# Causal masks taken off TensorE, and the order of a head's products redone, in a kernel of attention and two routed expert layers

## What is computed

```python
scores = scale * np.matmul(q, k.transpose(0, 1, 3, 2))
cum = np.cumsum(np.log(np.clip(f, 0.0001, 1.0)), axis=-1)
decay = cum[:, :, :, None] - cum[:, :, None, :]
causal = np.triu(np.ones((S, S), dtype=bool), k=1)
scores = np.where(causal, -1000000000.0, scores + decay)
scores = scores - np.max(scores, axis=-1, keepdims=True)
attn = np.exp(scores)
attn = attn / (np.sum(attn, axis=-1, keepdims=True) + 1e-09)
return np.matmul(attn, v)
```

## Time and profile before

| | us |
|---|---|
| three executions, median | 980.33 |
| lowest, highest of the three | 976.04, 981.48 |
| the profiled execution | 977.94 |
| its span | 976.4 |
| TensorE busy in the span | 905.9 |
| VectorE, ScalarE, Pool busy in the span | 554.5, 403.2, 229.0 |

### The profile page before, as it was taken

How to read it: one execution, slowest core, us unless ns; L and a number is a source line. 1 busy time by engine, 2 the same in 40 slices (tenths; PEclk the granted TensorE clock), 3 DMA queues, 4 the chain that set the end, 5 groups by cost and what they waited for, 6 DMA issues and landing times.

```text
span 976.4 us, 16405 instructions
## 1 busy us (share of the span) xinstructions
PE 905.9 (93%) x5244; PEld 727.0 (74%) x5245; DVE 554.5 (57%) x1524; ACT 403.2 (41%) x708; POOL 229.0 (23%) x287
## 2 busy tenths in 40 slices
PE   3999999999988859999999999995999999999996
PEld 3777677677666648888888888874888888888885
DVE  7565567557647526757567776752666243626633
ACT  1344444444445405525435543420555242525532
POOL 3111121321311242322232332313122212222211
PEclk9899999999979969999999999996999999999998
DMA  2334333444423019526254555421666124616110
GB/s 74 106 98 115 101 88 111 121 130 133 116 83 107 26 57 320 175 91 210 66 175 137 172 179 174 143 88 33 207 207 215 44 82 165 202 42 209 44 33 22
DMA packets 59242, 119.64 MB, mean 123 GB/s; under 512 B 11934, under 2 KB 20638, under 8 KB 59204
## 3 DMA queue, kind: packets, MB, share of 16 engines
q1 hardware_dynamic: 49476, 96.90, 31.5%
q0 software_dynamic: 9440, 22.18, 7.0%
q10 hardware_dynamic: 288, 0.07, 0.0%
HBM read 104.14 MB, written 17.99 MB: 125 GB/s over the span
## 4 chain that ended last, share of the span: by engine, by line
PE 86%; ACT 4%; DVE 4%; issue 2%; DMA 2%; POOL 1%; POOLq 0%; SPq 0%; DVEq 0%; ACTq 0%
PE ps L583 25%; PE ps L554 25%; PE ps L411 7%; PE ps L424 7%; PE ps L419 4%; PE ps L374 3%; PE ps L377 3%; PE ps L391 3%; PE ps L392 2%; PE ps L429 2%; ACT qB L626 2%; PE ps L379 1%; PE ps L401 1%; PE ps L395 1%; ACT o_rows L634 1%
## 5 line engine op out<-in xcount | busy, mean ns | idle before, releaser
L971 DVE TENSOR_TENSOR wlo<-stage,whi 128x1024 fp32r<-128x1024 f32 x136 | 160.0, 1221 | 35.7 <-ACT whi L651 34.1
L651 ACT CAST whi<-stage 128x1024 fp32r<-128x1024 f32 x136 | 133.7, 1056 | 0.1
L715 ACT ACTIVATE h_s<-ps 128x512 f32<-128x512 f32 x44 | 26.3, 599 | 224.1 <-PE ps L554 224.1
L620 ACT ACTIVATE probT<-ps 128x576 f32<-128x576 f32 (+4 forms) x160 | 66.2, 434 | 124.2 <-PE ps L395 111.4
L411 PE MATMUL ps<-probT,v_s 128*65 128x448 f32 (+4 forms) x384 | 111.1, 400 | 0.0
L554 PE MATMUL ps<-whi,xT_hi 128*128 128x512 f32 x352 | 96.9, 398 | 3.0 <-DVE xT_lo L1025 3.0
L583 PE MATMUL ps<-whi,hT_hi 128*128 128x512 f32 x352 | 99.5, 404 | 0.0
L583 PE MATMUL ps<-whi,hT_lo 128*128 128x512 f32 x352 | 99.2, 403 | 0.0
L554 PE MATMUL ps<-wlo,xT_hi 128*128 128x512 f32 x352 | 96.4, 396 | 0.0
L554 PE MATMUL ps<-whi,xT_lo 128*128 128x512 f32 x352 | 96.2, 396 | 0.0
L583 PE MATMUL ps<-wlo,hT_hi 128*128 128x512 f32 x352 | 94.9, 391 | 0.0
(11 more groups left out here) (175 smaller groups left out, 1566.0 us busy)
## 6 DMA issues: line engine op xcount, KB each, us to landing
stage<-in_moe_w SPq DMA_DIRECT2D x128, 512.0 KB, 3.8
q_raw<-in_q SPq DMA_DIRECT2D x64, 144.0 KB, 3.0
k_raw<-in_k SPq DMA_DIRECT2D x64, 144.0 KB, 3.1
v_s<-in_v SPq DMA_DIRECT2D x32, 162.5 KB, 2.3
x<-o_rows SPq DMA_DIRECT2D x8, 512.0 KB
kB<-cum_hl SPq DMA_DIRECT2D x64, 2.2 KB, 1.7
table<-entry POOLq DMA_INDIRECT x44, 2.1
table<-tinit SPq DMA_DIRECT2D x2, 288.0 KB
```

Of the source, the lines that this page charges most:

```text
L620: act.activation(probT[0:M, PT_AT[t]:PT_AT[t] + S - t * P], ps[0:M, T_AT[t]:T_AT[t] + S - t * P], ACT.Exp, scale=-1.0).then_inc(exps_done, 1)
L651: act.copy(whi[b][:, c, :], stage[:, c, :]).then_inc(w_hi[c], 1)
L971: dve.tensor_tensor(wlo[b][:, c, :], stage[:, c, :], whi[b][:, c, :].bitcast(F32), ALU.subtract).then_inc(w_lo[c], 1)
```

## The change

The query side's mask goes into the minimum: `tensor_reduce` becomes `tensor_tensor_reduce`, which adds a slice of a 128x576 float32 tile `maskf` (zero but for a triangle of 1e9 at its end) to the scores in PSUM, writes the sum back in place and gives the minimum as its accumulator. The key side's mask is dropped from TensorE; behind each exponential Pool sets the part above the diagonal of the block of `probT` to zero (`clear`, five selects per head), and `weighted` waits for `cleared` in place of `exps_done`. The orders of TensorE, VectorE, ScalarE and Pool within a head are rewritten. SyncE's list is not touched.

```diff
 def by_query(h, j):
-    diag = lo <= q0 < hi
-    ... identb[:], maskb[:, 0:M] ...
+    pe.matmul(o, qB..., kB..., start=True, stop=False)
+    mm = pe.matmul(o, qA..., kA..., start=False, stop=True)
 for h in range(HEADS):                      # TensorE
                 by_key(h, 0)
                 by_key(h, 1)
-                if h > 0:
-                    pe.wait_ge(ot_done, h)
-                    pe.wait_ge(s_embn, 3)
-                    back(h - 1)
                 if more:
                     operands(n)
                     by_query(n, 4)
                 pe.wait_ge(exps_done, QT * h + 1)
                 by_key(h, 2)
+                    by_query(n, 3)
                 pe.wait_ge(v_in[h % 3], (h // 3 + 1) * 16)
+                if h > 0:
+                    pe.wait_ge(ot_done, h)
+                pe.wait_ge(cleared, QT * h + 1)
                 weighted(h, 0)
                 by_key(h, 3)
                     by_query(n, 2)
                 pe.wait_ge(exps_done, QT * h + 2)
-                weighted(h, 1)
                 by_key(h, 4)
                     by_query(n, 1)
                     by_query(n, 0)
-                pe.wait_ge(exps_done, QT * h + 3)
-                weighted(h, 2)
+                pe.wait_ge(cleared, QT * h + 2)
+                weighted(h, 1)
+                if h > 0:
+                    back(h - 1)
                     minima_row(n)
+                weighted(h, 2)
+                weighted(h, 3)
+                weighted(h, 4)
                 if h % H == 6 and h > H:
+                    pe.wait_ge(norm_done, h)
                     g_ranks(h // H - 1)
-                weighted(h, 3)
-                weighted(h, 4)
 def mins(h, j):
-                dve.tensor_reduce(smin[0:q1 - q0, j:j + 1], ps[0:q1 - q0, S_AT[j]:S_AT[j] + q1], AX.X, ALU.min)
+                tile = ps[0:M, S_AT[j]:S_AT[j] + q1]
+                dve.tensor_tensor_reduce(out=tile, in0=tile, in1=maskf[0:M, at:at + q1], scale=1.0, scalar=LARGE,
+                                         op0=ALU.add, op1=ALU.min, accum_out=smin[0:M, j:j + 1])
 for h in range(HEADS):                      # VectorE
-                if h > 0:
-                    norm(h - 1)
-                    mins(n, 4)
                     leading_k(m)
+                    mins(n, 4)
                     mins(n, 3)
+                    rest_k(m)
                     mins(n, 2)
-                    rest_q(m)
                     mins(n, 1)
                     mins(n, 0)
-                    rest_k(m)
+                    rest_q(m)
+                    norm(h - 1)
+def clear(h, t):                            # Pool
+    block = probT[0:M, PT_AT[t]:PT_AT[t] + M]
+    pool.wait_ge(exps_done, QT * h + t + 1)
+    pool.affine_select(out=block, in_=block, compare_op=ALU.is_ge, fill=0.0, ...).then_inc(cleared, 1)
 for h in range(HEADS):                      # Pool
-                    copies(h + 2)
+                    copy_k(h + 2)
+                clear(h, 0)
+                clear(h, 1)
+                clear(h, 2)
+                    copy_q(h + 2)
+                clear(h, 3)
+                clear(h, 4)
```

More of the change, by code:

```diff
@@ L16 @@
 MASKED = 1.0e9
+LARGE = 3.0e38
 OOB = 1 << 20
-S_PASSES = 2
 def attention_moe_moe(nc, q_t, k_t, v_p, f, emb_t, tau, w1a, w2a, wg, w1b, w2b, out):
@@ L133, in attention_moe_moe @@
         probT = asb("probT", [P, PT_AT[-1] + LR])
+        maskf = asb("maskf", [P, S])
         smin = asb("smin", [P, QT], F32R)
@@ L489, in _ @@
                 by_key(h, 2)
+                if more:
+                    if h == 0:
+                        pe.wait_ge(s_embn, 1)
+                    if h > 1:
+                        pe.wait_ge(norm_done, h - 1)
+                if h % H == 7 and h > H:
+                    pe.wait_ge(rank_read, h // H)
+                if more:
+                    by_query(n, 3)
                 pe.wait_ge(v_in[h % 3], (h // 3 + 1) * 16)
+                if h > 0:
+                    pe.wait_ge(ot_done, h)
+                pe.wait_ge(cleared, QT * h + 1)
                 weighted(h, 0)
@@ L493, in _ @@
                 if more:
-                    if h > 0:
-                        pe.wait_ge(norm_done, h)
-                    by_query(n, 3)
                     pe.wait_ge(mins_done, QT * n + 1)
@@ L505, in _ @@
                     by_query(n, 0)
-                pe.wait_ge(exps_done, QT * h + 3)
-                weighted(h, 2)
+                pe.wait_ge(cleared, QT * h + 2)
+                weighted(h, 1)
+                if h > 0:
+                    if more:
+                        pe.wait_ge(mins_done, QT * (n + 1))
+                    pe.wait_ge(s_embn, 3)
+                    if h > 1:
+                        pe.wait_ge(norm_done, h - 1)
+                    back(h - 1)
                 if more:
@@ L817, in mins @@
                 q0, q1 = Q_TILES[j]
-                dve.tensor_reduce(smin[0:q1 - q0, j:j + 1], ps[0:q1 - q0, S_AT[j]:S_AT[j] + q1], AX.X,
-                                  ALU.min).then_inc(mins_done, 1)
+                M = q1 - q0
+                tile = ps[0:M, S_AT[j]:S_AT[j] + q1]
+                at = S - P + M - q1
+                dve.tensor_tensor_reduce(out=tile, in0=tile, in1=maskf[0:M, at:at + q1], scale=1.0, scalar=LARGE, op0=ALU.add,
+                                         op1=ALU.min, accum_out=smin[0:M, j:j + 1]).then_inc(mins_done, 1)
             def embeddings():
@@ L1111, in _, with copy_q, copy_k @@
             pool.sem_inc(s_pool, 1)
-            def copies(h):
-                a = h % 3
+            def copy_q(h):
                 pool.wait_ge(q_hi, h + 1)
-                pool.tensor_copy(qB[a][0:D, :], qA[a][0:D, :].bitcast(F32)).then_inc(q_cp, 1)
+                pool.tensor_copy(qB[h % 3][0:D, :], qA[h % 3][0:D, :].bitcast(F32)).then_inc(q_cp, 1)
+            def copy_k(h):
                 pool.wait_ge(k_hi, h + 1)
-                pool.tensor_copy(kB[a][0:D, 0:S], kA[a][0:D, 0:S].bitcast(F32)).then_inc(k_cp, 1)
-            copies(0)
-            copies(1)
+                pool.tensor_copy(kB[h % 3][0:D, 0:S], kA[h % 3][0:D, 0:S].bitcast(F32)).then_inc(k_cp, 1)
+            def clear(h, t):
+                M = min(P, S - t * P)
+                block = probT[0:M, PT_AT[t]:PT_AT[t] + M]
+                pool.wait_ge(exps_done, QT * h + t + 1)
+                pool.affine_select(out=block, in_=block, compare_op=ALU.is_ge, fill=0.0, base=0, pattern=[[1, M]],
+                                   channel_multiplier=-1).then_inc(cleared, 1)
+            for h in range(2):
+                copy_q(h)
+                copy_k(h)
             pool.iota(tok_i[:], pattern=[[S, B], [P, QT]], base=0, channel_multiplier=1)
```

41 lines of the change are left out of this document (14 added, 27 removed).

## The result

| | before | after |
|---|---|---|
| median of four executions, us | 979.23 | 1004.02 |
| lowest, highest | 976.04, 981.48 | 998.8, 1007.07 |
| the profiled execution, its span | 977.94, 976.4 | 998.8, 997.2 |
| mean granted clock in it | 0.964 | 0.934 |

The changed kernel is slower: the ratio is 1.024, with a 95% interval of 1.0199 to 1.0281. The forecast was 1014 us and slower, with a range of 988 to 1040.

What follows compares the result with a forecast made beforehand. TensorE's own instruction list, with its waits, was taken to bound the attention. Terms -28.5 + 37.1 + 17.5 + 5.7 + 6 - 3.5 = +34.3 on 977.9 gave 1012, 1014 us against the median; range 988 to 1040.

Steps and rivals of the forecast that it cites:

- the seven waits: TensorE before weighted 0 at h = 4, 8, ..., 28: late store delays k's load; 7 x 5.3 = +37.1 us.
- plain heads: TensorE, attention heads without special work: 8.97 us falls to 8.05 (7.9 to 8.3); 31 x 0.92 = -28.5 us.
- the clock behind them: TensorE after each 5.3 us idle: half clock for 3 to 6.8 us; 7 x 2.5 = +17.5 us.
- routing and its clock: Iteration ends at hh = 5 and 6: choose_batch and ranks come later; +5.7 us, plus +6 for lowered clock.
- squares, last batch: Heads behind squares wait about 0.4 instead of 0.68; two dear last-batch heads stay near 13 us; together -3.5.
- the mask's price: Ten mask matmuls per head on TensorE, by starts: five at 0.04, five at about 0.055, saving 0.49 us.
- The order's part: TensorE at a head's end: covered idle 0.28, last-minimum wait 0.1, and the last products' tail covered, giving 8.05 us.
- VectorE was in time: VectorE's last minimum ends at 5.6 us of the head, level with TensorE's 5.63, when `back` needs it.
- That the clock stays up: Rival: TensorE's clock stays up behind long waits, or saving and waits nearly equal; 991 us, chance 0.11.
- That the loads are in time: Rival: q and k loads arrive in time, leaving plain saving, routing and squares; 954 us, chance 0.13.
- That the minimum runs at half rate: Rival: VectorE's minimum with mask takes twice the time, a head takes 9.35 us; 1055 us, chance 0.08.
- The slowing of `rest_k` beside Pool: VectorE's `rest_k` between minima, blocked by Pool, could be 0.3 us late per head, 9 us in sum; median says nothing.

Runs made afterwards that it cites:

- the masks alone: Kernel before with minimum-with-mask on VectorE and selects on Pool, but TensorE, VectorE and ScalarE orders as before: 974.05 us, ratio 0.9939.
- the order alone: Changed kernel with masks back on TensorE as matmuls, plain reductions, no selects, new orders kept: 1004.88 us, ratio 1.0264 to the kernel before.
- Filling the waits: Changed kernel with 96 unused bf16 matmuls in front of the waiting weighting in the seven heads behind a store: 986.28 us, ratio 1.0067.
- the first: Changed kernel with SyncE's store and its wait for norm_done moved behind the q and k loads of head h + 3: 938.96 us, ratio 0.9592.
- the second experiment: Kernel before with SyncE's store and its norm_done wait moved behind the q and k loads: 978.48 us, ratio 1.0002.
- k-first: Changed kernel with both halves of k loaded before both halves of q within a head: 992.62 us, ratio 1.0132 to the kernel before.
- the last experiment: Changed kernel with the store behind the loads, Pool's copy of k behind the selects and VectorE's rest_k behind the minima: 934.79 us, ratio 0.9552.

## Why the prediction was right

The direction, the mechanism and each of its links held; the time was 10 us above the median measured, and the change 13.5 us above that between the two profiled executions. Term by term, against these (measured values are differences of the row copy's starts; the seven waits are the store heads' 61.5 less the clock's 21.0, the estimate above, and less 0.8 of excess that these heads had before):

| term | forecast | measured |
|---|---|---|
| plain heads | -28.5 | -44.6 |
| the seven waits | +37.1 | +39.7 |
| the clock behind them | +17.5 | +21.0 |
| routing and its clock | +11.7 | +10.0 |
| squares, last batch, first head | -3.5 | -4.2 |
| outside the attention | 0 | -1.0 |
| sum, before rounding | +34.3 | +20.8 |

That the total came so near is in part luck: the gain of the plain heads was forecast 16.1 us too small and the waits with their clock 6.1 us too small, and the two work against each other.

**The plain head is the term that was mis-sized.** 31 x 1.44 = 44.6 instead of 31 x 0.92. Of the 1.44, the masks are 0.90 and the order 0.54, if the order is changed first; the other way round the masks alone gave 0.33. The step that failed is the mask's price, 0.49 us per head, taken from its start to the next instruction's start. (Five at 0.04 and five at 0.055 are 0.475, not 0.49, which changes nothing.) That misses what the mask does behind it: the next product takes 0.22 us to its successor instead of 0.13, as shown with the order alone. The trace of before held it already: the product behind the mask starts at 102.20 and its successor at 102.42, while a product of the same width without a mask in front of it starts at 104.48 and its successor at 104.61. The mean duration of 234 ns would have been 2.3 us per head, far too much; what was right, 0.09 in the mean, lies between. The order's part was forecast at 0.43 (the covered end, the last minimum, the products' tail) and is 0.54.

**VectorE was in time, barely.** The last read-out begins at 103.48 and ends at 103.62, and `back` starts at 103.74, as close as the forecast had them (5.6 and 5.63 of the head; here 5.08 and 5.20). The read-out is 142 ns, of the 0 to 200 allowed. The masks alone, in an order with less room for the last minimum, show what it costs when that is not so: 0.5 us in nearly every head.

**The waits.** The forecast was 5.3 us; the place shown has 5.72, and the seven have 5.5 in the mean. All offsets of the chain were near: `norm` 6.51 us into the head (6.95), the store 7.68 (8.13), the load's 3.25 behind the store exactly, the cast 14.17 (14.48), the weighting 1.57 behind the cast (1.52). The difference is the shorter head: TensorE is ready for the weighting 10.0 us behind the first head's start instead of 10.7, and Pool is done with it only 0.26 us earlier than forecast. A faster TensorE waits longer for the same transfer.

**The clock.** 2.5 us per wait was taken between 1.5 and 3.4, from three waits of the last batch. Filling the waits gave back just that, 2.5 in the mean, but the agreement is partly chance: single places gave back 0.8 to 3.7, and with the later loads counted it is 1.8 or 3.9, 3.0 in the mean. The long kind goes beyond the 3.4 that the forecast allowed. That the clock stays up fell with the windows (0.50 from 111 to 117).

**The rivals.** That the loads are in time fell with the cast's row (6.41 us of waiting), and the first, second and k-first experiments show the load as the cause. That the minimum runs at half rate fell with 764 against 756 ns. The Trainium skill ("Vector Engine (DVE) Microarchitecture Reference", Points that are easy to get wrong) limits its rule to two SBUF sources that aren't bf16; here one is in PSUM, and the trace shows full rate. The slowing of `rest_k` beside Pool was allowed 9 us. The row of `rest_k` is 809 ns instead of 750, 0.06 per head and off the path: the nine didn't come.

**The range.** The terms given for the range add up to 22 us down and 20 up, so 992 to 1034 and not 995 to 1038. The bounds used, 988 to 1040, are wider than either, and what was measured is within all of them.

**The rest.** Each head's excess over the plain one, by the same differences of starts: the six heads around the routing of two batches went from 0.9 to 10.9 us, about what the forecast gave them with their clock (its 11.7 has the third batch in it too, whose head is in the next row here). Two errors cancelled in that row. The six heads with squares went from 2.8 to 4.7 us: with two squares a head has 0.83 instead of 0.68, where the forecast had 0.4, since the exponentials behind the squares are on the path, and one has 1.70, with the clock still at 0.50 from the wait before it. The two dear heads of the last batch take 9.3 instead of 13.8, where the forecast left them near 13. Most of that is the clock: before, it stood at 0.50 behind a wait in the first of them and from 285 to 290 us in the second. With the same products and the store moved (the second experiment) it stood at 1.00 from 269 to 290, and the two heads took 10.59 each. So 3.2 of the 13.8 is the clock's share, which the changed kernel doesn't have there (1.00 from 301 to 311), and the other 1.3 is near the 1.44 of a plain head. The forecast had put these heads down to the exponential.

## What to carry to other kernels

When a producer is moved to a later place, follow everything that is issued behind its wait, through each queue, up to the next engine that needs it: here a `norm` moved by four microseconds held up a store that stands in front of four loads, and cost some 60 us, where the store's place in SyncE's list makes a gain of 40 out of it. Do it for every operand that the queue carries: freeing the way of k alone showed the one of q behind it. And the price of a small matmul between large ones is read from two products start to start, with it and without it, not from its own start to the next.

## What the runs showed of the hardware

**Pool's cast beside VectorE's subtraction.** Pool's cast of q (64x576, SBUF to SBUF) takes 687 ns before and 1143 ns after, though nothing in it changed. Groups by shape on Pool, first after, then the order alone (no selects), then with both edits of the last experiment:

```profile
L1118 POOL CAST qB<-qA 64x576 fp32r<-64x576 f32 x32 | 36.6, 1143 | 17.1 <-ACT qA L614 17.1
```

```profile
L1125 POOL CAST qB<-qA 64x576 fp32r<-64x576 f32 x32 | 34.9, 1089 | 65.3 <-ACT qA L624 65.3
```

```profile
L1118 POOL CAST qB<-qA 64x576 fp32r<-64x576 f32 x32 | 21.9, 684 | 20.2 <-ACT qA L615 20.2
```

In the changed kernel it runs from 101.74 on beside `rest_k` (101.63, 0.74 long), a subtraction with two inputs in SBUF. It is slow without selects as well, and fast again where `rest_k` stands elsewhere. Where k is prepared behind the minima the slow one is the cast of k, 1129 ns, and that of q takes 695. The Trainium skill ("SBUF — State Buffer", Who interferes with whom) says that such an instruction of VectorE and one of GpSimd that reads SBUF block each other; the traces agree in kind. The size here is 0.46 us on Pool, whose cast started second, with a far smaller one on VectorE (809 against 750 ns).

**The clock falls within a wait.** At the place shown it was at 0.50 some 2.4 us into the idle time of 5.7 us, and stood there for 3.5 us of work behind it. Behind waits of nearly the same length (5.0 to 6.1 us) it stood there for 3.5 to 4 us of work in three places and for 11 to 12 in four. The head lost 1.8 us in the one case and 3.9 in the other, and a wait cut by 1.37 us could cost more than it gave.
